# Token mixing: one V product per tile instead of two, and the last batch's U products placed between its output projections

## The reference, cut to what matters

```python
xt = x.transpose(0, 2, 1)
h = xt @ U @ V                     # U: 576 x 32, V: 32 x 576
u = x + h.transpose(0, 2, 1)
ch = np.maximum(u @ w_ch1, 0.0) @ w_ch2
return (u + ch).astype(np.float32)
```

## Time and profile before

| | us |
|---|---|
| median of 3 runs (lowest, highest) | 1219.75 (1219.63, 1221.89) |
| the profiled execution's own time | 1217.24 |
| its span, first to last instruction | 1215.5 |
| PE busy | 1149.0 |
| DVE, ACT, POOL busy | 661.1, 542.1, 507.2 |

### The profile page before, as it was taken

The page is one execution under the profiler, slowest core; times in us unless marked ns, Lnnn a source line. Parts: engine busy times, 40 slices in busy tenths (PEclk is TensorE's granted clock), DMA queues, the critical chain, the costliest instruction groups (busy, mean ns, idle before and its releaser), DMA issues. The chain is left out here.

```text
span 1215.5 us, 19536 instructions
## 1 busy us (share of the span) xinstructions
PE 1149.0 (95%) x7232; PEld 956.4 (79%) x7232; DVE 661.1 (54%) x1497; ACT 542.1 (45%) x1131; POOL 507.2 (42%) x482
## 2 busy tenths in 40 slices
PE   6999999999999999978898989879999999999998
PEld 4777777777777777758777778569898989899896
DVE  4778888777788777746555656654120212112120
ACT  4666666566666666535565656634020201111010
POOL 5788899998888888742232323210000000000000
PEclk9999999999999999989999999999999999999999
DMA  7111122211111211030000001123000101010000
GB/s 200 53 53 50 53 60 60 59 56 54 50 51 58 60 59 40 21 135 4 1 2 18 23 18 49 40 91 113 27 26 1 53 1 52 0 52 0 26 1 26
DMA packets 47559, 54.56 MB, mean 45 GB/s; under 512 B 10992, under 2 KB 29424, under 8 KB 46960
## 3 DMA queue, kind: packets, MB, share of 16 engines
q1 hardware_dynamic: 47472, 53.42, 14.3%
HBM read 43.97 MB, written 9.44 MB: 44 GB/s over the span
## 5 line engine op out<-in xcount | busy, mean ns | idle before, releaser
L545 DVE TENSOR_REDUCE part_max<-psA 128x1 f32<-128x384 f32 x480 | 258.8, 557 | 76.4 <-PE psA L331 58.5
L496 ACT ACTIVATE pT<-psA 128x576 f32<-128x576 f32 x288 | 187.4, 652 | 167.8 <-PE psA L350 162.3
L249 POOL TENSOR_TENSOR pT<-pT 128x576 f32<-128x576 f32 x160 | 229.2, 1432 | 27.1 <-ACT pT L496 6.0
L331 PE MATMUL psA<-kT,qT 128*128 128x384 f32 x480 | 181.6, 392 | 12.5 <-DVE part_max L545 8.2
L364 PE MATMUL psA<-pT,v_raw 128*64 128x288 f32 x1152 | 153.8, 412 | 0.0
L1584 ACT ACTIVATE hid_hi<-psC 128x384 fp32r<-128x384 f32 x96 | 47.2, 492 | 197.4 <-PE psC L1509 197.3
L341 PE MATMUL psA<-qT,kT 128*128 128x288 f32 x576 | 133.0, 313 | 0.4 <-ACT pT L496 0.4
L1603 DVE SCALAR_TENSOR_TENSOR hid_lo<-psC,hid_hi 128x384 fp32r<-128x384 f32 x96 | 53.5, 558 | 136.6 <-ACT hid_hi L1584 136.6
L331 PEld LDWEIGHTS psA<-kT,qT 128*128 128x128 f32 x480 | 89.8, 192 | 46.7 <-DVE part_max L545 30.4
L350 PE MATMUL psA<-qTm,kT 128*128 128x288 f32 x576 | 123.4, 296 | 0.2 <-ACT qTm L482 0.2
L364 PEld LDWEIGHTS psA<-pT,v_raw 128*64 128x64 f32 x1152 | 77.0, 136 | 53.3 <-issue 6.7
(11 more groups left out here) (158 smaller groups left out, 1931.4 us busy)
## 6 DMA issues: line engine op xcount, KB each, us to landing
k_raw<-in_k SPq DMA_DIRECT2D x32, 288.0 KB, 3.0
v_raw<-in_v SPq DMA_DIRECT2D x32, 288.0 KB, 2.8
q_raw<-in_q SPq DMA_DIRECT2D x32, 256.0 KB, 3.3
w_raw<-in_moe_w_ch SPq DMA_DIRECT2D x1, 4096.0 KB, 13.7
u_rows<-x_all SPq DMA_DIRECT2D x16, 256.0 KB, 2.0
w_raw<-in_moe_w_ch SPq DMA_DIRECT2D x16, 256.0 KB, 2.7
u_first<-u_rows SPq DMA_DIRECT2D x3, 768.0 KB, 4.5
u_second<-u_rows SPq DMA_DIRECT2D x3, 768.0 KB, 4.7
```

The source lines that it names most:

```text
L249: nc.gpsimd.tensor_tensor(pT[:, KT, :], pT[:, KT, :], pT[:, j, :], ALU.add).then_inc(part_summed, 1)
L331: nc.tensor.matmul(maxes[n % 2][:, 0:PIECE], qT[h % 3][:, t * P:(t + 1) * P], kT[u][:, c * PIECE:(c + 1) * PIECE], start=True, stop=True). ...
L496: nc.scalar.activation(pT[:, j, :].rearrange("p (a c) -> p a c", a=2), scores[n % 2][:, :, 0:HALF], ACT.Exp, scale=0.5 * float(D) ** -0.5) ...
L545: nc.vector.tensor_reduce(part_max[u][:, t, c:c + 1], maxes[n % 2][:, 0:PIECE], AX.X, ALU.max).then_inc(max_freed[n % 2], 1)
```

## The change

- `V4` is one tensor: the four copies of V are cast to hi, then copies 1 and 3 (rows 32 to 63 and 96 to 127) are overwritten by the lo part, one POOL instruction each. So `split_V` has three instructions (128 x 576, then twice 32 x 576) where it had two.
- Behind "down", ACT copies PSUM rows 64 to 127 (the odd tiles' sum) to `mixed_odd`; DVE adds rows 0 to 63 to it, giving `mixed_sum`, and frees the bank; ACT casts the sum to rows 0 to 63 of `mixed`; DVE writes the lo part to rows 64 to 127. ACT and DVE wait for each other at each of these.
- `mix_out` is one product per tile, of all 128 rows.
- In the last batch, U's products of tiles 0 and 1 stand behind wo 2, that of tile 2 behind wo 3, that of tile 3 behind wo 4, and that of tile 4 in the place of "down".

```diff
-        ops.tensor_copy(self.V4[0][:, :], self.V4_raw[:, :]).then_inc(done, 1)
-        pool.wait_ge(done, at + 1)
-        split_lo(ops, self.V4[1][:, :], self.V4_raw[:, :], self.V4[0][:, :]).then_inc(done, 1)
-        pool.wait_ge(done, at + 2)
+        ops.tensor_copy(self.V4[:, :], self.V4_raw[:, :]).then_inc(done, 1)
+        for n in range(2):
+            rows = slice((2 * n + 1) * self.RANK, (2 * n + 2) * self.RANK)
+            pool.wait_ge(done, at + n + 1)
+            split_lo(ops, self.V4[rows, :], self.V4_raw[rows, :], self.V4[rows, :]
+                     ).then_inc(done, 1)
+        pool.wait_ge(done, at + 3)
...
+    DOWN_BEHIND = {2: (0, 1), 3: (2,), 4: (3,)}
...
-            def mix_down(b):
+            def mix_down(b, tiles):
-                wait_freed(b, [("wo", t) for t in range(QT)], ("down",))
+                wait_freed(b, [("wo", t) for t in tiles], ("down",))
                 out = claim(b, ("down",))
-                for t in range(QT):
+                for t in tiles:
...
-                mm.then_inc(filled, 1)
+                if tiles[-1] == QT - 1:
+                    mm.then_inc(filled, 1)
...
                 if t == 0:
-                    wait_freed(b, [("down",)], use)
+                    pe.wait_ge(mix_ready, b + 1)
                 out = claim(b, use)
-                for w in range(2):
-                    mm = nc.tensor.matmul(out[0:rows, :], V4[w][:, span(t)], mixed[:, :],
-                                          start=(w == 0), stop=(w == 1))
-                mm.then_inc(filled, 1)
+                nc.tensor.matmul(out[0:rows, :], V4[:, span(t)], mixed[:, :], start=True,
+                                 stop=True).then_inc(filled, 1)
...
                     project_out(b, use[1])
+                    if b == batches - 1 and use[1] in DOWN_BEHIND:
+                        mix_down(b, DOWN_BEHIND[use[1]])
                 elif kind == "down":
-                    mix_down(b)
+                    mix_down(b, range(QT) if b < batches - 1 else [QT - 1])
...
-                    ins = split_hi(nc.scalar, mixed[:, :], src[:, :])
+                    nc.scalar.activation(mixed_odd[:, :], src[P // 2:P, :], ACT.Copy
+                                         ).then_inc(mix_copied, 1)
+                    act.wait_ge(mix_summed, b + 1)
+                    ins = split_hi(nc.scalar, mixed[0:P // 2, :], mixed_sum[:, :])
...
+            def mix(b):
+                use = ("down",)
+                src, of_bank = staged(b, use)
+                dve.wait_ge(mix_copied, b + 1)
+                nc.vector.tensor_tensor(mixed_sum[:, :], src[0:P // 2, :], mixed_odd[:, :],
+                                        ALU.add).then_inc(mix_summed, 1)
+                dve.wait_ge(mix_summed, b + 1)
+                dve.sem_inc(of_bank, 1)
+                dve.wait_ge(hi_done, hi_no[b, use] + 1)
+                split_lo(nc.vector, mixed[P // 2:P, :], mixed_sum[:, :], mixed[0:P // 2, :]
+                         ).then_inc(mix_ready, 1)
...
-                elif kind == "down":
-                    for r in (RANK, 3 * RANK):
-                        ins = split_lo(nc.vector, mixed[r:r + RANK, :], src[r:r + RANK, :],
-                                       mixed[r:r + RANK, :])
```

More of the change, by code:

```diff
@@ L656, in __init__ @@
         self.wo_s = [sb(f"wo_{n}", [P, E * HD // P, DM], F32R) for n in ("hi", "lo")]
-        self.V4 = [sb(f"V4_{n}", [P, self.SQ], F32R) for n in ("hi", "lo")]
+        self.V4 = sb("V4", [P, self.SQ], F32R)
         self.U2 = sb("U2", [P, self.QT, 2 * self.RANK])
@@ L721, in split_V @@
         pool.wait_ge(done, at)
-        ops.tensor_copy(self.V4[0][:, :], self.V4_raw[:, :]).then_inc(done, 1)
-        pool.wait_ge(done, at + 1)
-        split_lo(ops, self.V4[1][:, :], self.V4_raw[:, :], self.V4[0][:, :]).then_inc(done, 1)
-        pool.wait_ge(done, at + 2)
-    SPLITS = 26
+        ops.tensor_copy(self.V4[:, :], self.V4_raw[:, :]).then_inc(done, 1)
[5 more added lines that the diff above has]
+        pool.wait_ge(done, at + 3)
+    SPLITS = 27
 def experts(nc, ready, x_all, x_ready, ident, u_rows, u_saved, batches, w1, w1_stays, load_u):
@@ L821, in experts @@
         yT = [sb(f"yT_{n}", [P, YC, SQ], F32R) for n in ("hi", "lo")]
+        mixed_odd = sb("mixed_odd", [P // 2, DM])
+        mixed_sum = sb("mixed_sum", [P // 2, DM])
         mixed = sb("mixed", [P, DM], F32R)
@@ L871, in experts @@
         pe_passed = sem("b_pe_passed")
+        mix_copied = sem("mix_odd_copied")
+        mix_summed = sem("mix_summed")
+        mix_ready = sem("mix_ready")
         padded = sem("k_lo_padded")
@@ L1365, in do @@
                     invert(batches * STEPS - 1)
-                if has_parts(use):
+                if use[0] == "down":
+                    mix(b)
+                elif has_parts(use):
                     lo_of(b, use)
```

## The result

| | before | after |
|---|---|---|
| median, us (lowest to highest, runs) | 1219.69 (1219.05 to 1221.89, 4) | 1227.88 (1227.10 to 1228.61, 4) |
| profiled execution: its own time, span | 1217.24, 1215.5 | 1228.27, 1226.5 |

The changed kernel is slower: ratio 1.0063, 95% interval 1.0044 to 1.0082, 8.2 us between the medians. The forecast was 1221.4 with a range to 1224.2, so the time lies outside it. A second measurement on another chip gave the same (1.0061, 1.0047 to 1.0075).

What follows compares the result with a forecast made beforehand. PE was taken as the bound on average, with POOL setting the pace in attention heads 8 to 15. Terms +1.5 - 0.5 + 0.7 = +1.7 us gave a median of 1221.4 us, range 1218.2 to 1224.2.

Steps and rivals of the forecast that it cites:

- Part 1: Attention, heads 8 to 15: POOL's added 32-row subtraction passes on to PE one for one, +1.5 us.
- Parts 2 and 3: Experts' steps, batches 0 to 2: fewer V products (-0.92, -0.23) and down's longer chain (+0.65), together -0.5 us.
- Part 4: Last batch's end: moved U products and ACT's weight cast delay the odd copy; the MLP starts later, +0.7 us.
- A change between array forms: Last batch's end: PE switching between full and half array loses record overlap, 0.1 us each, 0.4 us for four.
- The rival that was priced too low: Half clock behind PE's longer stall in head 15: +1.5 us, 1222.9 us, chance 0.28; at the MLP's start some tenths.

Runs made afterwards that it cites:

- v_third_op: The kernel before plus one redundant POOL operation (32 rows x 576) behind V's split in attention: 1222.48 against 1217.57 us, ratio 1.0033.
- warm: The changed kernel with 34 unused products filling PE's waits at the last batch's end (25 behind down, 9 behind u 4): 1224.39 against 1219.75 us, ratio 1.0039.
- best_old: The kernel before with POOL's 26 preparing instructions one per head and 7 and 5 unused products in PE's waits: 1208.18 against 1219.53 us, ratio 0.9907.
- sum_in_psum: The changed kernel with DVE's sum of both halves kept in down's PSUM bank, not SBUF: 1224.23 against 1217.57 us, ratio 1.0049.
- spread: The changed kernel with POOL's 27 preparing instructions done one per head in heads 5 to 31: 1216.30 against 1219.75 us, ratio 0.9965.
- before_again: The kernel before, unedited, measured and traced a second time: 1219.68 against 1219.53 us, ratio 1.0000.
- v_twice_last: The changed kernel with each of the last batch's five V products issued twice: 1227.38 against 1219.75 us, ratio 1.0064.

## Why the prediction was wrong

**Part 1, V's split: right.** 1.5 us were forecast; A is longer by 1.5, and by 1.2 beyond that only in v_third_op. The two subtractions on 32 rows took 3.31 us, 1.66 each, between the 1.42 and 1.83 of the same operation on 128 rows. The wait of L563 was 2.86 us (forecast 2.8), PE's stall 2.69 (forecast 2.7).

**Parts 2 and 3, batches 0 to 2: the mechanism right, the sum overlaid.** In the changed kernel's first trace each step's distance from the same step before shows the added delay behind down as 0.56 us in all three batches (forecast 0.65); in batches 0 and 1 it is gone at the next step, in batch 2 it stays, and PE's wait there grew from 0.58 to 1.13:

```profile
771.14 0.76 PE L1071 MATMUL psB<-moe_kT,moe_qT 128*64 128x512 f32 x4 [1.13 <-ACT moe_probs L1248]
```

u 0 gave 0.23 in each batch, u 1 only 0.05 where it was to give 0.23. Traces with the same number of stretches at half clock agree: 3 stretches, 219.0 and 218.9 without the new mixing, 219.0 and 218.7 with it. Warm and the kernel before have their 3 stretches in the same steps, and there the new mixing ends 0.3 us ahead. An exception is best_old, with 3 stretches and 220.0. So the parts are worth between nothing and -0.3, where -0.5 was forecast. What moved S by up to 3.4 us are those stretches, near 1 us each. The changed kernel had 6 of them in both its traces, but 3 in sum_in_psum and warm, which are the same program up to the last step but for where the sum lies. The granted clocks of the single runs speak against the change as the reason. On one chip they are 0.9810 on average over five runs of the changed kernel and 0.9865 over fifteen of the kernel before. By twice the missing share of the span, an estimate, that is some 14 us more at half clock per run. The MLP's start alone has 17.1 us at half clock in both traces of the changed kernel, and 3.4 and none in those before. That leaves nothing for S: its 2.2 us belong to the profiled executions, and the medians, 8.2 us apart, hardly have them. By what the stretches fall stays open.

**Part 4, the end: the step that failed.** The prediction gave "copy 0.60, sum 0.69, cast 0.60, lo 0.69 and handovers". The lo part took 3.16. I had the duration of DVE's subtractions from rows in which one operand lies in PSUM, and I had POOL's split of the last weight beside them, but only asked which of the two ends last. Of the lo parts of `mixed` the new one is the first that reads both operands from SBUF. Beside POOL's instruction it doesn't run, it waits for that to end: 3.16 and 1.94 us, both to 0.55 us after POOL's end, and 0.69 when POOL starts later or when one operand is in PSUM. That is 2.5 us of the 3.9 in E.

The rows on record already had this price, and I overlooked it. DVE's L563 reads both operands from SBUF too. It took 0.76 us in later heads, where POOL was idle, and 1.97 in head 15, where this instruction of POOL had just begun:

```profile
283.00 1.42 POOL L216 TENSOR_TENSOR k_parts<-k_raw,k_parts 128x576 fp32r<-128x576 f32 x1
```

L563 ended at 285.04, 0.62 us after POOL's 284.42. In both places that is 0.14 less than the instruction takes alone (0.76 and 0.62, 0.69 and 0.55). The Trainium skill (SBUF — State Buffer, SBUF: two separate sides) states this as an exclusive lock: a DVE operation with two SBUF inputs and a GpSimd operation share a pair of ports, and whichever starts first has it for its whole instruction. These rows agree. One row of spread does not: L560, the same instruction as L563, took 0.77 us from 118.30 on, within a scaling of POOL (L697) that ran from 117.56 to 118.91.

The rest of Part 4 came out as forecast. The forecast was worked out from one trace, and against that trace E grew by 3.2: 2.5 of the lo part and 0.7 as forecast, with ACT's weight cast in front of the odd copy. The mean of E says 3.9, since E is 26.8 in before_again; with that spread the close agreement may be luck. A change between array forms was priced at 0.1 us, and the first cost 0.09: U's first product started at 794.48, where the next product of the same form was due at 794.39. That the trace before agreed with a full loss of the overlap was a wrong reading: there, from wo 3 on 128 columns to wo 4 on 64 (790.80 and 0.63, then 791.27), the overlap is the usual 0.16.

**The rival that was priced too low: the second step that failed.** Half clock was a rival in attention, with its place wrong; for the MLP's start I wrote "some tenths", and the sum has nothing for it. It cost 1.0 us in M and 2.4 in F. In all eight traces in which PE's gap in front of u 0 was 2.6 us or more and nothing filled it, the MLP began at half clock or fell to it within 0.8 us; of three with a gap of 2.1, one did; of the three that filled it, none. My own sum implied a longer gap (from 2.1 to about 3.4: down's end near 796.6, u 0 at 799.95), and I didn't carry it on to what comes after it. That PE's idle time at the last batch's end is the cause is shown by warm. How the cost divides between the wait in front of u 0, which grew by 3.8 us, and the one behind u 4, which grew by 0.4, is not shown.

Together: 1.5 of A, 3.9 of E and 3.4 of M and F are 8.8 us, and 8.3 with the -0.5 between A and S. The medians are 8.2 apart. Luck has a small part in that: E and S of single traces vary by more than the difference.

## What to carry to other kernels

Price an elementwise instruction of DVE by where its operands lie, not by its shape alone: one that reads both from SBUF must not stand beside a long GpSimd subtraction on a path where it counts; one instruction that takes 1.97 us in one place and 0.76 in another, in the trace that one has, is the sign to look for. Work taken off TensorE in front of a dense stage is worth nothing if waits take its place: here, unfilled gaps of 2.6 to 5.9 us were followed by 2.1 to 3.8 us lost at half clock in M and F. Either shorten the chain of engines that makes the gap, or fill it. And look for the engine that sets the pace of each stage: spreading POOL's preparation over the heads brought attention's end 11 us forward in the changed kernel and 8 to 10 in the kernel before, more than any edit of the mixing.

## What the runs showed of the hardware that was not expected

- A DVE subtraction of 64 x 512 with both operands in SBUF took 0.69 us alone and 3.16, 3.27 and 1.94 us beside GpSimd's subtraction of 128 x 2048; with one operand in PSUM it took 0.69 beside it. A DVE addition of 128 x 576 took 0.76 alone and 1.97 beside a GpSimd subtraction, but 0.77 within a GpSimd scaling.
- TensorE stayed at half clock for 17 us (804.1 to 821.1) of the changed kernel, the last 4 of them busy throughout.
- In v_twice_last it came back to full clock for 3.4 us and fell again, with PE busy for 1.35 of these and no wait longer than 2.0 us.
- 34 unused matmuls of 128 x 512 in waits took both losses behind them away (M and F 3.24 and 33.57 instead of 4.21 and 35.61), about 3 us of the kernel.
